# Another order for the last two token tiles and the first expert's gather in a retention + mixture-of-experts kernel

## The reference, cut to what matters

```
q, k, v: (2, 8, 768, 64)      x = attn_out as (1536, 512)
state = gamma[h] * state + k_t v_t^T          # per head, in order of time
y_t   = q_t state / sqrt(64)

logits = x @ w_gate                            # 8 experts, capacity 384
expert_idx = argmax(logits, axis=1)
for i in range(1536):                          # tokens queue up at their expert
    e = expert_idx[i]
    if counts[e] < capacity: disp[e, counts[e]] = x[i]; pos[i] = counts[e]; counts[e] += 1
h = relu(disp @ w1)  (512 -> 1024);  y = h @ w2  (1024 -> 512)
out[i] = gate_w[i] * y[expert_idx[i], pos[i]]

h = x @ w_in (512 -> 2048); g = P(h) / (Q(h) + 1e-6); result = g @ w_out
```

## Time and profile before

| | us |
|---|---|
| median of 3 runs | 536.94 (536.67 to 537.17) |
| the profiled execution | 536.65 |
| its span (first to last instruction) | 534.8 |
| PE busy | 525.8 (98%) |
| DVE / ACT / POOL busy | 423.5 / 329.6 / 76.4 |
| granted TensorE clock | 1.00 throughout (the upper of its two levels) |

### The profile page before, as it was taken

One profiled execution on the slowest core, in us unless ns is written; L12 is line 12 of the kernel. 1 busy time (PEld: TensorE's weight loads), 2 busy tenths in 40 slices (PEclk: granted clock), 3 DMA queues, 4 the chain that ended last, 5 costly groups with the idle time before them and its releaser, 6 DMA issues.

```text
span 534.8 us, 8739 instructions
## 1 busy us (share of the span) xinstructions
PE 525.8 (98%) x3209; PEld 439.0 (82%) x3209; DVE 423.5 (79%) x759; ACT 329.6 (62%) x508; POOL 76.4 (14%) x74
## 2 busy tenths in 40 slices
PE   6999999999999999999999999999999999999997
PEld 4888888888888888888788888888888888888885
DVE  2578788785856759577989999997888888787886
ACT  2464546584655747457969867658566566655652
POOL 3343342260101101003010010004000000200000
PEclk9999999999999999999999999999999999999999
DMA  9999959959968384903060000003000000200002
GB/s 194 232 247 254 275 199 392 396 147 389 380 237 303 149 332 144 398 29 99 23 217 1 1 21 20 1 1 113 7 21 20 1 0 1 80 1 0 0 1 79
DMA packets 65087, 72.26 MB, mean 135 GB/s; under 512 B 41234, under 2 KB 41746, under 8 KB 65044
## 3 DMA queue, kind: packets, MB, share of 16 engines
q1 hardware_dynamic: 58596, 57.96, 34.5%
q0 software_dynamic: 3136, 9.46, 5.2%
q10 hardware_dynamic: 3312, 4.28, 2.3%
HBM read 59.09 MB, written 12.60 MB: 134 GB/s over the span
## 4 chain that ended last, share of the span: by engine, by line
PE 96%; DMA 1%; DVE 1%; SPq 1%; issue 0%; ACT 0%
PE up_low L949 7%; PE up_low L950 7%; PE up_low L951 7%; PE bank L949 6%; PE bank L950 6%; PE bank L951 6%; PE up_high L955 6%; PE up_low L955 5%; PE yrows L949 4%; PE yrows L950 4%; PE up_high L951 4%; PE up_high L949 4%; PE up_high L950 4%; PE yrows L951 4%; PE up_high L956 3%; PE up_low L956 3%
## 5 line engine op out<-in xcount | busy, mean ns | idle before, releaser
L876 DVE TENSOR_TENSOR T<-raw,T 128x1024 fp32r<-128x1024 f32 x60 | 71.5, 1219 | 33.8 <-ACT T L870 33.8
L870 ACT ACTIVATE T<-raw 128x1024 fp32r<-128x1024 f32 x60 | 60.5, 1070 | 32.2 <-PE bank L951 31.8
L949 PE MATMUL up_low<-x2H,T 128*128 128x512 f32 x176 | 69.3, 394 | 0.0
L951 PE MATMUL up_low<-x2H,T 128*128 128x512 f32 x176 | 68.5, 389 | 0.0
L950 PE MATMUL up_low<-x2L,T 128*128 128x512 f32 x176 | 68.5, 389 | 0.0
L1529 ACT ACTIVATE sq<-up_low 128x512 f32<-128x512 f32 x44 | 26.2, 596 | 64.4 <-PE up_low L951 64.1
L1550 DVE SCALAR_TENSOR_TENSOR wa<-sq,coef,wa 128x512 f32<-128x512 f32 x48 | 35.9, 748 | 28.7 <-ACT wa L1531 28.7
L949 PE MATMUL bank<-T,hL 128*128 128x512 f32 x128 | 50.6, 395 | 0.0
L951 PE MATMUL bank<-T,hH 128*128 128x512 f32 x128 | 49.9, 390 | 0.0
L950 PE MATMUL bank<-T,hH 128*128 128x512 f32 x128 | 49.8, 389 | 0.0
L1543 ACT ACTIVATE rc<-wa,cst 128x512 f32<-128x512 f32 x48 | 34.8, 725 | 20.6 <-DVE wa L1550 15.9
(11 more groups left out here) (205 smaller groups left out, 1228.7 us busy)
## 6 DMA issues: line engine op xcount, KB each, us to landing
raw<-in_moe_w_dram SPq DMA_DIRECT2D x14, 2048.0 KB, 10.9
raw<-in_moe_w_dram SPq DMA_DIRECT2D x8, 512.0 KB, 5.1
w_out_raw<-in_moe_w_out_dram SPq DMA_DIRECT2D x4, 1024.0 KB, 17.1
ybuf<-ysb ACTq DMA_DIRECT2D x15, 256.0 KB
qin<-in_q_dram SPq DMA_DIRECT2D x12, 256.0 KB, 5.3
kin<-in_k_dram SPq DMA_DIRECT2D x12, 256.0 KB, 5.7
vin<-in_v_dram SPq DMA_DIRECT2D x12, 256.0 KB, 5.6
xbuf<-xt SPq DMA_DIRECT2D x12, 256.0 KB, 4.2
```

The costliest lines, as they stand in the source:

```text
L870: e.activation(W[w][:, 0, cols], raws[par][:, w, cols], ACT.Copy).then_inc(r.wH[w], 1)
L876: e.tensor_tensor(W[w][:, 1, cols], raws[par][:, w, cols], W[w][:, 0, cols].bitcast(F32), ALU.subtract).then_inc(r.wL[w], 1)
L949: nc.tensor.matmul(out_, aL, bH, start=start, stop=False)
L951: return nc.tensor.matmul(out_, aH, bH, start=False, stop=stop)
```

## The change

Nothing is added to the computation or taken from it; four engines get another order in the passage from tile 10 to the first expert. PE does tile 11's values right behind its query, then the logits and rows of tile 10 and of tile 11, then the positions of tile 10, and the late rows of expert 0 later. DVE copies the logits of tile 11 ahead of tile 10's place, and puts tile 9 in the table behind tile 11's choice. ACT copies y of tile 11 ahead of the rows of tile 10. POOL starts the two gathers ahead of tile 9's low part.

```diff
         def pe_last_tiles():
             t = NT - 1
             pe_query_state(t)
+            pe_values(t)
             pe_logits_apart(t - 1)
             pe_rows(t - 1)
             pe_logits_sum(t - 1)
-            pe_values(t)
-            pe_x_late(0, range(2))
-            pe_positions(t - 1)
-            pe_x_late(0, range(2, 3))
             pe_logits_apart(t)
-            pe_x_late(0, range(3, KD))
             pe_rows(t)
+            pe_positions(t - 1)
+            pe_x_late(0, range(2))
             pe_logits_sum(t)
+            pe_x_late(0, range(2, KD))
             pe_x_late(1, range(KD))
-            pe_index(t - 2)
-            pe_x_stored(range(2))
             pe_positions(t)
+            pe_x_stored(range(2))
             pe_x_stored(range(2, KD))
             pe_x_late(2, range(KD))
+            pe_index(t - 2)
             pe_index(t - 1)
...
             dve_choose(late + 1)
+            dve_logits_apart(late + 2)
             dve_place(late + 1)
             dve_fit(1)
             dve_count(late + 1)
-            dve_logits_apart(late + 2)
+            dve_choose(late + 2)
             dve_put(late)
-            dve_choose(late + 2)
...
-            pool_low_rows(0)
             pool_x_stored()
-            for i in range(1, LAST):
+            for i in range(LAST):
                 pool_low_rows(i)
...
-            for t in range(NT):
+            for t in range(NT - 1):
                 act_tile(t)
-            act_evac_xT(NT - 1)
-            act_rows(NT - 1)
+            for t in range(NT - 2, NT):
+                act_evac_xT(t)
+            for t in range(NT - 2, NT):
+                act_rows(t)
```

More of the change, by code:

```diff
@@ L701, in pe_last_tiles @@
             pe_logits_sum(t - 1)
-            pe_values(t)
+            pe_logits_apart(t)
+            pe_rows(t)
+            pe_positions(t - 1)
             pe_x_late(0, range(2))
-            pe_positions(t - 1)
-            pe_x_late(0, range(2, 3))
-            pe_logits_apart(t)
-            pe_x_late(0, range(3, KD))
-            pe_rows(t)
             pe_logits_sum(t)
+            pe_x_late(0, range(2, KD))
             pe_x_late(1, range(KD))
-            pe_index(t - 2)
+            pe_positions(t)
             pe_x_stored(range(2))
-            pe_positions(t)
             pe_x_stored(range(2, KD))
             pe_x_late(2, range(KD))
+            pe_index(t - 2)
             pe_index(t - 1)
```

## The result

The changed kernel takes **539.12 us** (median of 14 runs, 537.9 to 542.66) against 537.12 (median of 14 runs of the kernel before, on the same chip): ratio 1.0039, interval 1.0027 to 1.0052. The forecast was 538.2 with a range up to 538.6; it had the direction and the mechanism inside the passage, but the median lies above the range. The profiled execution is 538.28 with a span of 536.4; that of before was 536.65 and 534.8.

The account below looks back on a forecast made before the run. PE, busy 525.8 of 534.8 us, was taken as the bound, so only its waits count. Order 0.0, DVE hold +1.38 and gather -0.1 gave +1.28 on 536.65, plus 0.29 to the median: 538.2, range 536.7 to 538.6.

Parts of the forecast that it names:

- the mechanism inside the passage: Tile 10 to first expert: POOL's low parts hold short DVE instructions, so PE waits for tile 10's positions; 1.38 us.
- the sum: Whole kernel: order 0.0, hold +1.38, gather -0.1, together +1.28 on 536.65; with 0.29 to the median, 538.2.
- slower: Whole kernel: the verdict that the time lies beyond the 0.2% bound at 538.0; chance 0.41.
- the turned rows behind tile 11's positions: PE, from tile 11's positions to the last late rows: 0.06 and then 2.00 us.
- rival (4): POOL's gathers start behind 70, tile 9's low part ends near 73.5, hold certain; 538.2 to 538.4; chance 0.50 with full hold.
- the 0.55 that the order alone was to leave: PE ahead of tile 10's positions: a wait of some 0.55 us from the new order without any hold.
- The gain of 0.1 on the gather of expert 1: L913 behind the passage: an earlier gather landing no longer delays PE; 0.1 us gained, range 0 to 0.2.
- the new order alone is worth 0.0: PE's passage without holds: the 0.55 wait eats the saved entries and gaps; last late rows at 78.25 against 78.27.
- (1): Rival, DVE beside POOL's low parts: nothing is held where it matters; 536.8, no slower; chance 0.24.
- (2): Rival: tile 10's choice 0.1 to 0.25 late, `fit` or tile 11's choice held; 0.2 to 0.5, 537.2; chance 0.22.
- (b): Tile 10's low part on POOL, 73.70 to 74.98, holds L520; choice ends 75.01, last late rows 1.38 later.
- (3): Rival, whole kernel: a gain from saved PE gaps, the gather and earlier weights; 536.2 at best; chance 0.04.

Follow-up runs that it names:

- e5: Changed kernel with each of POOL's low parts made by four instructions of 128 columns instead of one of 512; 539.75 us, ratio 1.0012, on the second chip.
- e9: Changed kernel with tile 9's low part again ahead of the gathers and every low part in four pieces of 128 columns; 537.65 us, ratio 1.0013.
- e6: The changed kernel again, no edit, on the second chip; 540.85 us, ratio 1.0036.
- e1: Changed kernel with POOL's old order alone put back, tile 9's low part ahead of the two gathers; 538.32 us, ratio 1.0021.
- e8: The changed kernel once more, no edit, for another profile on the second chip; 541.28 us.
- e12: Kernel before with the gathers ahead of tile 9's low part and PE's waits left open, on the third chip; 541.6 us.
- e14: The changed kernel with no edit, its wait left open, as pair of e13 on the second chip; 540.2 us, ratio 1.0043.
- e10: Kernel before with gathers ahead of tile 9's low part and PE's two waits filled by 3 and 6 matmuls of zeros; 539.19 us.
- e13: Changed kernel with seven matmuls of zeros in PE's wait ahead of tile 10's positions, on the second chip; 538.69 us, ratio 1.0013.
- e3: Changed kernel with seven matmuls of zeros in PE's wait ahead of tile 10's positions, on the first chip; 538.27 us, ratio 1.0019.
- e4: Changed kernel with tile 9's table matmul (L408) moved ahead of the last late rows; 539.99 us, ratio 1.0062.
- e2: Kernel before with only POOL's two gathers moved ahead of tile 9's low part, on the first chip; 541.6 us, ratio 1.0093.
- e7: Changed kernel with tile 9's lane (L541, L545, L547) moved behind tile 11's choice on DVE, second chip; 541.3 us, ratio 1.0052.

## Why the prediction was right and wrong

**What was right.** The values of tile 11 were forecast at about 70.5 and begin at 70.59; tile 10's logits near 71.5, at 71.61. The choice of tile 10 was to end at 75.01 with POOL's second low part, with positions at 75.07: it ends at 75.11, and positions begin at 75.17. The last late rows were forecast at 79.65 and begin at 79.47; the loop near 84.2, and it begins at 83.99. On tile 10's choice the end was right and the shares were not: L520 was to take about 1.1 and takes 0.54, because most of the delay is already in L547; both end with POOL's second low part, and that is what set the time. The runs at a full clock have a median of 538.19, and the sum said 538.2. That agreement is in part luck: in the profile behind it (538.28) the passage is 1.06 longer and not 1.38, and the landing costs 0.44 where 0.1 was to be gained. e5 and e9 show the cause by the size of POOL's pieces: L520 falls from 1.22 (e6) to 0.23 (e5), L535 from 1.24 (e1) to 0.41 (e9).

**The step that failed: the clock was taken as given.** The prediction read the granted clock of 1.00 off the profile of before and carried it over, while forecasting a new idle time of about 1.7 us on PE. No term, rival or bound stood for what an idle PE does to its own clock. Half of the 14 runs have a lower mean clock. None of those 7 was profiled; in the profiles of e8, e12 and e14 the clock fell to 1.2 GHz for 3.4 to 6.8 us, 0.6 to 0.7 us behind the end of the wait or, in e14, within it. One fall of 3.4 us costs 1.4 in the pair e10 and e12. Such falls lift the median by 0.9 (539.12 against the 538.19 of the runs at a full clock), out of a range that ended 0.4 above the forecast. Filling the wait with useless matmuls takes nearly all of the low clocks away (2 of 26 runs are left) and leaves the passage as long as it was (14.00 and 14.01 on one pair of profiles, 14.94 and 14.94 in e6 and e13). The range's upper end should have had one fall of the clock in it, and with it "slower" deserved more than 0.41.

**Terms that were off.** The passage is 1.06 to 1.2 longer, depending on whether one starts at the query or at the span's beginning, where 1.38 was forecast: the term that was mis-sized is that of the turned rows behind tile 11's positions, which take 1.85 to the last late rows (77.62 to 79.47) where 0.06 and 2.00 were put. The gathers were to start at 69.23 and start at 70.09: behind an idle time of 4.35 the first begins 0.9 after its index, where 0.17 was taken from a row without such an idle time. That is the condition of rival (4), and the hold that it made certain is what happened: the low part ended at 73.78, not at 72.9 to 73.1. PE's wait was to be about 1.7 and is 1.39, and the 0.55 that the order alone was to leave is 0.24 in e1: L373 of tile 10 still takes 0.31 to the next row (72.46 to 72.77), where 0.14 was put, so PE's own work ends later. The gain of 0.1 on the gather of expert 1 may be there, but is no larger than the scatter: the distance from the loop to L912 is 8.32 to 8.34 in e1, e3, e4 and e13 and 8.86 in the first profile, 8.42 and 8.55 in the two of before. Last, "the new order alone is worth 0.0" is by e9 a bound rather than a value: 0.38 or less, and near 0 by the estimate above.

**The rivals.** (1) falls: L520 was not ahead of POOL's second low part. (2) has a true core that (b) had too: the hold is not tied to one instruction but falls on L547, L520, L566 or L535, whichever of them stands beside a low part, and e1 shows it best, where the freed choice only passed the hold on to the count. (3), a gain, has nothing for it in any run.

**What stays open.** Why the clock falls in some runs of one kernel and not in others, and more than once or for longer in some: a mean of 0.989 over 540.9 us is some 12 us at the lower level, an estimate from the two levels. Why e5 has 7 low runs of 12 with a wait of 0.8 only; the kernel before had 6 of 24 on that chip in the same comparison, so the chip has a part in it. And why the kernel before takes 0.9 to 1.6 us more on that chip; all profiles from it, all of the changed kernel or its variants, show PE's L373 waiting 0.8 us for a late copy of the logits.

## What to carry to other kernels

Where GpSimd runs a tensor_tensor, look at which small VectorE instruction stands beside it and who is queued behind that; putting one such pair right may only pass the hold to the next (e1), and shorter GpSimd instructions shorten every hold at once (e5). Whenever a change adds an idle time to an engine that was busy throughout, write a term for its clock into the sum and the range. And when a kernel's runs fall into groups, read the mean clock of each run before explaining the median: the median of the changed kernel is neither of its two groups.

## What the runs showed of the hardware

- Waits of TensorE of 1.23 to 1.52 us went with the lower clock level for 3.4 to 6.8 us in e8 and e12 (0.7 and 0.6 us behind the end of the wait) and e14 (0.4 us ahead of it), the three executions with the wait open that were profiled at a mean clock of 0.997 or less; the same waits in the profiles of after, e2, e4, e6 and e7 came without it.
- VectorE's hold can outlast one GpSimd instruction: a comparison of 3 elements stood for 3.14 us through two low parts of 1.25 (e2, e10, e12), while in the changed kernel L547 came free between the first and the second. It was due 0.6 us ahead of POOL's recorded start of the low part in e2; what decides between the two isn't known.
- VectorE's L511, L513, L515 and L518 kept 0.15, 0.16, 0.23 and 0.16 us beside a running low part (73.73 to 74.53 in the changed kernel), as elsewhere; L547, L520, L566 and L535 were held. So L520, for which no row of before spoke, is held like L547, and L545 with its one element is not (0.27 at 72.56, and 0.27 at 78.19 with POOL idle).
- Of the held instructions one is a sum of two bf16 operands of 8 elements in SBUF (L535, 1.24 against 0.15). The Trainium skill, SBUF — State Buffer, SBUF: two separate sides, counts a VectorE instruction with two SBUF inputs among those that need the shared ports against a GpSimd instruction that reads SBUF; the trace agrees.
- An indirect DMA of GpSimd behind an idle time of over 4 us began 0.9 after its index was written (70.09 against 69.19).
